# Dense stage in blocks of 512 tokens with a last one of 256

## The reference

```python
def _moe_ref(x, w_in, w_out):            # w_in 512x2048, w_out 2048x512
    h = x @ w_in
    g = h * (1.0 / (1.0 + np.exp(-1.702 * h)))
    return g @ w_out
def _moe2_ref(x, w_gate, w1, w2):        # 8 experts, F = 1024
    logits = x @ w_gate
    expert_idx = np.argmax(logits, axis=1)
    ...                                   # gate_w: softmax weight of the chosen expert
    for e in range(E):
        mask = expert_idx == e
        h = np.maximum(x[mask] @ w1[e], 0.0)
        out[mask] = gate_w[mask, None] * (h @ w2[e])
```

## Time and profile before

| | |
|---|---|
| median of 3 runs | 779.75 us (779.72 to 780.51) |
| the profiled execution: its own time | 780.57 us |
| its span, first to last instruction | 778.4 us |
| PE busy | 761.2 us (98%) |
| DVE / ACT / POOL busy | 352.5 / 321.1 / 335.5 us |
| granted TensorE clock, mean | 0.996 |

### The profile page before, as it was taken

The page is one execution under the profiler, slowest core; times in us unless marked ns, Lnnn a source line. Parts: engine busy times, 40 slices in busy tenths (PEclk is TensorE's granted clock), DMA queues, the critical chain, the costliest instruction groups (busy, mean ns, idle before and its releaser), DMA issues.

```text
span 778.4 us, 15793 instructions
## 1 busy us (share of the span) xinstructions
PE 761.2 (98%) x5508; PEld 709.4 (91%) x5509; DVE 352.5 (45%) x902; ACT 321.1 (41%) x722; POOL 335.5 (43%) x290
## 2 busy tenths in 40 slices
PE   8999999999999999999999999999999999999994
PEld 7888888999999899899899889999999999999994
DVE  6887877211244334424424446465862332332231
ACT  4888888432422332233233223253324325325220
POOL 6798982352222232222213232244527627438421
PEclk9999999999999999999999999999999999999998
DMA  8887881120500010020020001511172613420121
GB/s 339 288 280 289 279 289 32 41 69 0 190 1 1 20 61 0 0 81 0 0 81 0 0 0 42 200 49 41 31 258 91 208 55 124 158 61 30 30 62 32
DMA packets 25733, 74.17 MB, mean 95 GB/s; under 512 B 3153, under 2 KB 4049, under 8 KB 25569
## 3 DMA queue, kind: packets, MB, share of 16 engines
q1 hardware_dynamic: 22000, 63.09, 23.2%
q0 software_dynamic: 3264, 10.03, 4.2%
q10 hardware_dynamic: 432, 0.59, 0.2%
HBM read 61.11 MB, written 12.58 MB: 95 GB/s over the span
## 4 chain that ended last, share of the span: by engine, by line
PE 87%; POOL 3%; DVE 2%; DMA 2%; issue 2%; ACT 1%; POOLq 0%; SPq 0%; DVEq 0%; ACTq 0%
PE pj L734 26%; PE nm L916 17%; PE kv L916 8%; PE pj L1361 8%; PE kv L1408 7%; PE nm L1408 7%; PE nm L1361 5%; PE pj L268 2%; DMA qk<-in_qk_n 2%; PE kv L284 2%; PE nm L346 1%; PE pj L1421 1%; POOL sqt L211 1%; PE tr L1357 1%; POOL sqt L215 1%
## 5 line engine op out<-in xcount | busy, mean ns | idle before, releaser
L890 POOL TENSOR_TENSOR gl<-g,gh 128x384 fp32r<-128x384 f32 x96 | 98.1, 1023 | 294.3 <-ACT gh L752 294.3
L747 DVE TENSOR_TENSOR g<-pj,sg 128x384 f32<-128x384 f32 x96 | 53.4, 557 | 188.5 <-ACT sg L742 188.2
L734 PE MATMUL pj<-xh,win_h 128*128 128x384 f32 x384 | 129.2, 336 | 0.0
L734 PE MATMUL pj<-xh,win_l 128*128 128x384 f32 x384 | 128.9, 336 | 0.0
L734 PE MATMUL pj<-xl,win_h 128*128 128x384 f32 x384 | 128.6, 335 | 0.0
L742 ACT ACTIVATE sg<-pj 128x384 f32<-128x384 f32 x96 | 47.2, 491 | 140.0 <-PE pj L734 140.0
L752 ACT ACTIVATE gh<-g 128x384 fp32r<-128x384 f32 x96 | 50.5, 526 | 102.1 <-PE kv L916 64.6
L858 DVE SCALAR_TENSOR_TENSOR raw<-tr,xT 128x512 f32<-128x512 f32 x90 | 58.6, 688 | 34.7 <-ACT tr L810 29.1
L734 PEld LDWEIGHTS pj<-xh,win_h 128*128 128x128 f32 x384 | 72.1, 188 | 1.7
L734 PEld LDWEIGHTS pj<-xl,win_h 128*128 128x128 f32 x384 | 72.1, 188 | 1.6
L734 PEld LDWEIGHTS pj<-xh,win_l 128*128 128x128 f32 x384 | 72.0, 188 | 0.0
(11 more groups left out here) (274 smaller groups left out, 1687.2 us busy)
## 6 DMA issues: line engine op xcount, KB each, us to landing
wraw<-in_moe_w SPq DMA_DIRECT2D x7, 2048.0 KB, 10.7
ve<-in_v_z SPq DMA_DIRECT2D x16, 585.0 KB, 4.2
qk<-in_qk_n SPq DMA_DIRECT2D x15, 576.0 KB, 6.0
qkT<-in_qk_t SPq DMA_DIRECT2D x15, 576.0 KB, 6.6
y_rows<-ys SPq DMA_DIRECT2D x18, 256.0 KB, 2.4
stage<-in_moe_w_in SPq DMA_DIRECT2D x8, 512.0 KB, 6.4
y_early<-ys SPq DMA_DIRECT2D x12, 256.0 KB, 2.8
stage<-in_moe_w_out SPq DMA_DIRECT2D x4, 512.0 KB, 6.1
```

What stands on the lines that cost most here:

```text
L734: mm = eng.matmul(ph[f % 3][:, 0:BT], w[f // F1A][:, c, f % F1A, :], x[:, c, :], start=(c == 0 and w is win_h and x is xh), stop=(c == DC ...
L747: eng.tensor_tensor(g32[f % 2][:, :], ph[f % 3][:, 0:BT], sg[f % 2][:, :], ALU.mult).then_inc(v_g, 1)
L890: eng.tensor_tensor(gl[f % 3][:, :], g32[f % 2][:, :], gh[f % 3][:, :].bitcast(F32), ALU.subtract).then_inc(g_gl, 1)
```

## The change

`BT` becomes 512. There are four blocks of 512 tokens and a last one of 256: 4 x 4 tiles and 2. An `up` is 12 matmuls of 512 columns, in the last block of 256; a block of four tiles has 12 matmuls in a `down`, the last block 6. The matmuls are these before and after: 1152 ups and 864 downs, then 960 and 864.

Room for this is found as follows. The features are written over the sigmoid in `sg`, and `g32` goes; `sig` now waits for POOL's gl(f - 2) and `mul` no longer does. There are four `py` banks but only three `ys` buffers (`YS`): ACT copies tile 3 into ys0, after it has copied ys0 for the router and after the stores of the first three tiles have landed. The router's copy goes to the bank `pr`, in the last block to `py[2]`. The gate weights come in one DMA. The pairs of the router stand at other f (`PAIRS`), 16 per block. All four first blocks are stored to `y_early` too. The experts' small tiles and hTl, xTl, xb lie at other addresses; w1 of the first expert may be loaded as soon as the last block's x is split. The experts' steps in the last block move: PE's ranks to f = 3, `inverse_early` to 8, `rows` to 9, ACT's highs to f = 8, 9 and 12, 13; three of the four low parts of w1 go from DVE to POOL, at f = 11 to 13, the fourth stays with DVE at f = 13.

```diff
-BT = 384
-BLOCKS = N // BT
+BT = 512
 BK = BT // P
+BLOCKS = (N + BT - 1) // BT
+LAST_K = NT - BK * (BLOCKS - 1)
...
     def sig(eng, n, f):
+        at = slice(0, tiles_of(n) * P)
         eng.wait_ge(p_h, F1 * n + f + 1)
-        need(eng, v_g, F1 * n + f - 1)
-        eng.activation(sg[f % 2][:, :], ph[f % 3][:, 0:BT], ACT.Sigmoid, scale=1.702).then_inc(a_sg, 1)
+        need(eng, g_gl, F1 * n + f - 1)
+        eng.activation(sg[f % 2][:, at], ph[f % 3][:, at], ACT.Sigmoid, scale=1.702).then_inc(a_sg, 1)
...
-        need(eng, g_gl, F1 * n + f - 1)
-        eng.tensor_tensor(g32[f % 2][:, :], ph[f % 3][:, 0:BT], sg[f % 2][:, :], ALU.mult).then_inc(v_g, 1)
+        eng.tensor_tensor(sg[f % 2][:, at], ph[f % 3][:, at], sg[f % 2][:, at], ALU.mult).then_inc(v_g, 1)
...
-            need(eng, y_done, 16 * BK * n)
-            if not last:
-                need(eng, ye_done, 16 * BK * n)
-            for k in range(BK):
+            stored(n, 0)
+            for k in range(tiles_of(n)):
                 if last:
                     eng.wait_ge(p_yk, k + 1)
-                eng.activation(ys[k][:, :], py[k][:, :], ACT.Copy).then_inc(a_y, 1)
+                if k == YS:
+
+                    beside_logits(n, 0, isinstance(n, int) and n == BLOCKS - 2)
+                    eng.wait_ge(a_yp, BK * n + 1)
+                    stored(n, YS)
+                eng.activation(ys[k % YS][:, :], py[k][:, :], ACT.Copy).then_inc(a_y, 1)
...
         half(F1 - 2, 0)
-        half(F1 - 2, 1)
         beside["tensor"](eng, F1)
         half(F1 - 1, 0)
+        half(F1 - 2, 1)
+        beside["tensor"](eng, F1 + 1)
+        turn(0)
         half(F1 - 1, 1)
-        beside["tensor"](eng, F1 + 1)
-        half(F1 - 2, 2)
-        turn(0)
-        half(F1 - 1, 2)
         eng.wait_ge(ld_wg, 16)
-        turn(1)
...
         route(0)
-        turn(2)
+        turn(1)
+        for i in range(FILL):
+            beside["first_up"](eng, DC + i)
         route(1)
-        route(2)
...
-                eng.wait_ge(*dense["pairs"])
-                eng.wait_ge(*dense["early"])
+                for done in dense["stored"]:
+                    eng.wait_ge(*done)
                 gather(eng, 0)
+            if 11 <= f < 14:
+                low(eng, 0, 0, f - 11)
...
-            if 10 <= f < 14:
-                low(eng, 0, 0, f - 10)
+            if f == 13:
+                low(eng, 0, 0, CHUNKS - 1)
```

## The result

The changed kernel takes 792.69 us (median of six runs, 791.14 to 793.67), beside 779.89 for the kernel before on the same chip (779.28 to 780.7). The ratio is 1.0162, with a 95% interval of 1.0149 to 1.0175: slower. The forecast was 793.0 with a range of 786 to 799. The profiled execution took 791.14 us with a span of 789.2, so 10.8 us more span than before; it is the fastest of the six. The time is right; the terms behind it are not all right, and they erred in both directions.

A forecast was written before the change was run, and what follows sets the result against it. The prediction took the dense stage to be bound by PE. Gains of 2.3 and 1.3 us against waits and restarts summed to +12.7 on the profiled 780.57 us, 793.3, or 792.5 against the median; it said 793, range 786 to 799.

The forecast's parts named there:

- rival (b): Dense stage: the clock falls in the new idle stretches, +3 to +8 us, so 796 to 801; chance 0.15.
- PE's work: Dense stage and router: 192 matmuls fewer gain 2.3 us, the router's two tiles in place of three gain 1.3.
- Inner boundaries: Two inner block boundaries: up(3) waits for mul(0) behind the stores' landing and fourth copy, 0.3 to 0.4 each, 0.7 us.
- End of block 0: Boundary after block 0: the gate weights' load delays the stores behind it and so mul(0); 3.2 us.
- Last boundary: Start of the last block: its short ups make up(3) due at 4.3 us, mul(0) ends at 8.0; 3.7 us.
- ranks' 1.2 and down(1)'s 0.3: Last block: PE's ranks wait 1.2 us for DVE's early choice; mul(1) and gl(1) make down(1) late by 0.3.
- The gather: Last block: POOL issues the gather behind gl(10), holding gl(11) back 4.5 us, so down(11) waits 2.0 us.
- turn_x(1), gl(14) and the port: Last block: turn_x(1), gl(14) and two turns late, 2.0 us; DVE's and POOL's low parts meeting on the port, 1.0.
- Way out: End of the last block: cover for the router's turns gets shorter, waits of 0.6 and 0.5, 1.1 us.
- Restarts: After each of ten waits PE's first weight load is not hidden, 0.08 us each, 0.8 us.
- Rival (a): Only the block boundaries bind, POOL and ACT catch up in the last block; 787 us, chance 0.20.
- Rival (c): Block boundaries: the stores' landing no longer gates, everything in the last block is on time; -2.2, 778.4 us, chance 0.04.

The follow-up runs named there:

- e1: The changed kernel with ACT's fourth copy of ys moved from the block's end to behind high(1) of the next block; 782.27 us, ratio 1.0029.
- e3: The changed kernel with the gate weights' load issued behind the stores of block 0 instead of ahead of them; one run, 789.29 us.
- e4: The changed kernel with twenty unused 128x512 matmuls added on PE just before up(3) of the last block; 791.29 us, ratio 1.0139.
- e6: e5 with all four low parts of w1 on POOL, the last behind gl(14) instead of on DVE; 783.65 us, ratio 1.0045.
- e7: e5 with all four low parts of w1 on DVE at f = 10 to 13, none on POOL there; 782.86 us, ratio 1.0035.
- e2: The changed kernel with the fourth copy in place but waiting only for the landing of tile 0's two stores, not all six; 783.78 us, ratio 1.0048.
- e5: e1 with POOL issuing the gather behind gl(9) instead of gl(10); 781.01 us, ratio 1.0011.
- e8: The changed kernel with only the gather moved, behind gl(9) instead of gl(10); 789.33 us, ratio 1.0115.
- e9: e5 with ACT's four high parts of w2 at f = 10, 11, 11 and 12 instead of two each at 12 and 13; 780.57 us, ratio 1.0007.
- e11: e10 with the fourth copy behind high(2), POOL's w1 lows behind gl(11), gl(12), gl(14), gl(15), DVE's w2 lows behind the last yT copy; 778.6 us, ratio 0.9984.
- e10: e9 with down(12), down(13) ahead of turn_x(0), turn_x(1), and w1's low parts all on POOL, behind gl(11), gl(12) and gl(15); 784.42 us, ratio 1.0051.

## Why the prediction was right, and where it was not

Before, the first up starts at 133.56 and the late ranks at 545.25, 411.7 us apart; after, at 133.46 and 556.31, 422.9 apart. What follows the ranks is the same in both (their distance to PE's last matmul is 223.0 us in each). So all terms lie between, 11.2 us against the 12.7 forecast. The other five runs of the changed kernel are 1.3 to 2.5 us longer than this one, with a mean granted clock of 0.988 to 0.990 in place of 0.992. That is some 3 to 7 us more at the low level, which costs up to half as much (an estimate, from the shares and the span). So what brings the median to 12.8 may lie in more of rival (b); these runs have no trace.

**PE's work: mis-sized, the largest miss.** The sum gave -3.6 us. The waits and the slow stretch below add up to 17.5 (8.9 at the boundaries, 2.6, 0.6, 3.6, 1.1 and 0.7), so the work fell by 6.3. The step that failed is the rate: 228.9 ns for every matmul of 512 columns, for the ups after the change and for "The downs (864 of them) stay", taken from 18 downs between ups of 384. In the four big blocks of the changed kernel all are 512 wide, and a block of 384 matmuls takes the 87.04 us that e1's rows show, 226.7 ns each; four such blocks are 3.4 us less than the 87.9 each of the forecast. The prediction's sign of being wrong, that ups of 512 do not come at 229 ns, came about to this extent. With the 3.6 that makes 7.0. Of the 0.7 between, 0.5 lies in the kernel before: its blocks take 66.40 us, where the two rates give 66.48. The last block's two f take 5.62 us (505.39 to 511.01), the 2.81 each of the forecast. PE in the changed kernel at the change from up to down:

```profile
300.87 0.39 PE L753 MATMUL pj<-xl,win_h 128*128 128x512 f32 x1
301.10 0.39 PE L753 MATMUL pj<-xh,win_l 128*128 128x512 f32 x1
301.32 0.39 PE L950 MATMUL nm<-wb_h,gh 128*128 128x512 f32 x1
301.55 0.39 PE L950 MATMUL nm<-wb_l,gh 128*128 128x512 f32 x1
```

They come 0.22 to 0.23 apart with no step at the change.

**Inner boundaries: 0.7 forecast, 2.35 measured.** One waits 0.35 us as forecast, the other 2.0. There the last store took 4.5 us to land and not 2.8. (The terms that the prediction names add up to 8.44 us and not 8.6, a wait of 0.2; the same 0.15 is too much in its end of block 0. The 0.35 is thus met with a sum that is slightly off.) At the later of the two ACT's fourth copy starts 8.3 us into the block (399.73), where that of the block before started 6.65 us into it (318.85 less 312.20):
```profile
408.03 0.60 ACT L870 ACTIVATE ys<-tr 128x512 f32<-128x512 f32 x1 [5.75 <-DMA y_early<-ys]
```

**End of block 0: 3.2 forecast, 1.27 measured.** The mechanism held (e3), the size didn't. The step that failed is the load's landing: one DMA of 2 MB, which I gave the 8.8 us of the second of two, landed 7.1 after its issue (220.24 to 227.31), 3.55 us into the block and not 5.4.

**Last boundary: 3.7 forecast, 5.28 measured**, from 493.09 to 498.49 less the 0.12 of one matmul. Again the last landing, 4.4 us in place of 2.8.

**The clock (rival b): held at 0.15, came about at the last boundary.** The mechanism is told right, and it is shown by e4: +2.6 us on PE. It fell once and not twice. The sum had nothing for it. What the prediction cites of the Trainium skill (TensorE: Matmul & The Clock Gate, "HAM oscillation"), that idle gaps between groups of matmuls let the clock fall and the next group starts cold, is borne out in part: gaps inside a stage of matmuls brought it down in this kernel and in five of the experiments, but three of this kernel's four waits on mul passed without a fall. It hid the **ranks' 1.2 and down(1)'s 0.3**, which were 0 here and 0.6 for the ranks with the clock up (e4).

**The gather: 2.0 forecast, 0.5 to 0.6 measured at gl(11)**: down(11) was due 4.2 us after gl(10) and not 3.3, since PE was late from the boundary and the clock, and the gather held gl(11) back for 4.05 us (528.50 to 532.55) and not 4.5. With the boundaries silent it was 2.4 (e1). **turn_x(1), gl(14) and the port: 3.0 forecast together, 3.6 measured** (2.1, 1.3 and 0.2). The port's 1.0 was low. DVE and then POOL in the changed kernel:

```profile
536.10 3.74 DVE L1200 TENSOR_TENSOR W<-w_raw,W 128x1024 fp32r<-128x1024 f32 x1
...
541.33 2.50 DVE L1200 TENSOR_TENSOR W<-wraw,W 128x1024 fp32r<-128x1024 f32 x1
```
```profile
536.30 2.41 POOL L1200 TENSOR_TENSOR W<-w_raw,W 128x1024 fp32r<-128x1024 f32 x1
538.67 1.74 POOL L924 TENSOR_TENSOR gl<-sg,gh 128x256 fp32r<-128x256 f32 x1
...
542.71 1.69 POOL L924 TENSOR_TENSOR gl<-sg,gh 128x256 fp32r<-128x256 f32 x1
```

DVE's 3.74 in place of 1.22 is 2.5 us of waiting, and it works the other way too: gl(13) and gl(14) take 1.7 in place of 0.74. I had counted what DVE loses to POOL and nothing for what POOL loses to DVE. By the Trainium skill (SBUF — State Buffer, "Who interferes with whom") the order of issue decides which of the two is blocked, so either can be. The trace agrees in that both lose, but the order is less plain: the 3.74 us one starts at 536.10, 0.20 before POOL's subtraction and beside the end of gl(12) (535.61 to 536.37), and it still ends behind it. What the port costs the whole kernel no experiment tells by itself: e6 and e7 change the lists with it.

**Way out: 1.1 forecast, 1.1 measured** (0.67 and 0.41). **Attention: 0.3 forecast, none**: the first up starts 0.1 earlier, less than single traces differ by (133.2 to 134.4 in the fourteen traces). **Restarts: 0.8 forecast, about 0.7 measured**, 0.11 for the first matmul behind each wait.

In sum, the forecast landed within 0.3 us with +16.3 of costs and -3.6 of work where the trace has +17.5 and -6.3. That it is so near is in part luck: the clock's +2.6, which the sum left out, and the 2.7 of work that it missed cancel, and without the clock the costs are 14.9. Its direction and its main causes were right: e1 and e2 show them for the boundary, e5 and e8 for the gather, e9 for ACT's highs ahead of turn_x(1). Rival (a), that only the boundaries bind, is refuted by e8: the gather's place alone gave some 3.5 us. Rival (c), that nothing would bind and the time be 778.4, has the number that e11 reached with 778.6, but not by its terms: e11 takes the landing out of the way and lays the last block anew, and with 6.3 us less work it still waits for over 3.

## What to carry to other kernels

A buffer that is used again within the same step puts a DMA's landing into an engine's list. Before moving such a copy to the end of a block, ask what stands behind it there; one instruction moved four places on gave back 10.4 of 12.8 us. When a block is halved beside work of fixed size, the engines beside it become the bound, and then each engine's order is worth 1 to 3 us: pull what feeds the next stage forward, and keep long VectorE and GpSimd subtractions of SBUF tiles apart. Take a matmul's rate from the pattern of widths that the changed kernel will have: a rate read where two widths alternate was 1% too slow here for one width alone.

## What the runs showed that was not expected

**Matmuls of 512 columns come a little slower behind narrower ones.** Behind ups of 384 columns the nine matmuls of the first down come 224 to 236 ns apart and the nine of the second 226 or 227, 228.9 on average over the 18. In the changed kernel's last block, behind ups of 256, the six of the first down (from 508.26) take 231 each and the next six 227. With equal widths all are 226 or 227. Over the 1536 matmuls of the four big blocks, to which the forecast gave 228.9, 2.2 ns each make 3.4 us. Why they are slower no run shows.

**A single instruction fetch beside a landing.** The last store's landing took 4.5 and 4.4 us in exactly the two boundaries in which one packet of the kind "instruction" crossed the stores. The DMA view at the clean boundary and at one of these two:

```profile
DMA packets 864, 1.57 MB, mean 286 GB/s; under 512 B 96, under 2 KB 96, under 8 KB 864
q1 hardware_dynamic: 864, 1.57, 76.7%
```
```profile
DMA packets 865, 1.59 MB, mean 230 GB/s; under 512 B 96, under 2 KB 96, under 8 KB 864
q1 hardware_dynamic: 864, 1.57, 61.8%
q8 instruction: 1, 0.02, 0.8%
```

The stores are the same 864 packets. The fetch takes 0.93 us, and behind it the last packets of the stores come in one by one, 0.08 us apart, as from one of the sixteen DMA engines alone: 22 of them over 1.6 us at the last boundary (nine at the other), when all the others are done. The twelve experiments have the same: at these two boundaries, with one fetch each, the slowest y_early store lands 4.3 to 4.8 us after its issue, and at the boundary before them, with none, 2.9 to 3.0. That the fetch is the cause is argued from this coincidence; no kernel moved it to another boundary.

**How short a wait brings the clock down is not fixed.** It fell behind waits of 5.1 to 5.3 us (three traces) and 2.6 (e1), and in e8 behind one of 1.96 at the third boundary, where the changed kernel's own wait of 2.0 at the same place passed without a fall. It fell behind one of 1.9 in e6, and in e3 behind one of 2.1 at turn_x(1), which passed in the changed kernel. In e10 it fell behind waits of 0.67 and 1.75 us (by the starts of the matmuls) close together. In e7 a wait of 3.4 us passed without one. That a slow stretch need not cost time is the other half: in the changed kernel 2.6 us of it were covered by an engine that was late anyway.
